# ELU between two matmuls: the Relu on ScalarE is dropped, a two-step clamp is added on VectorE

## What is computed

```python
# 1. gated linear attention, 4 batches x 8 heads, 768 steps, head dim 48
S_re, S_im = a * (S_re, S_im) + (k v^T, 0)      # complex decay a per channel
y[t] = q[t] @ S_re
# 2. MLP with ELU: x is (3072, 384), w_in (384, 2048), w_out (2048, 384)
h = x @ w_in
g = np.where(h > 0.0, h, np.exp(np.minimum(h, 0.0)) - 1.0)
x = g @ w_out
# 3. MLP with a maximum of three: w1, w2, w3 (384, 768), w_fin (768, 384)
out = np.maximum(np.maximum(x @ w1, x @ w2), x @ w3) @ w_fin
```

## Time and profile before

| | |
|---|---|
| time, median of 3 runs | 925.01 us (924.41 to 926.62) |
| time of the profiled execution | 925.01 us |
| span in the profile, first to last instruction | 923.1 us |
| PE busy | 841.4 us, 91% of the span |
| PEld busy | 729.5 us, 79% |
| ACT busy | 478.1 us, 52% |
| DVE busy | 438.9 us, 48% |
| POOL busy | 365.7 us, 40% |
| mean granted TensorE clock | 0.981 |

### The profile page before, as it was taken

The page is one execution under the profiler, slowest core; times in us unless marked ns, Lnnn a source line. Parts: engine busy times, 40 slices in busy tenths (PEclk is TensorE's granted clock), DMA queues, the critical chain, the costliest instruction groups (busy, mean ns, idle before and its releaser), DMA issues.

```text
span 923.1 us, 14390 instructions
## 1 busy us (share of the span) xinstructions
PE 841.4 (91%) x5692; PEld 729.5 (79%) x5692; DVE 438.9 (48%) x606; ACT 478.1 (52%) x709; POOL 365.7 (40%) x272
## 2 busy tenths in 40 slices
PE   0057899999999999999999999999999999999997
PEld 0047799888887888788878888888888889898987
DVE  4857776866666666666757332333112121212120
ACT  6746776777768676868685635642121211211121
POOL 3543654453545454445454423555222131303120
PEclk9987899999999999999999999999999999999999
DMA  5397143636252524353433425002010102000000
GB/s 224 87 277 205 35 135 95 187 103 196 60 169 78 183 73 154 90 172 89 138 112 116 124 82 211 0 27 94 9 60 0 69 1 69 1 35 1 35 0 35
DMA packets 70723, 88.45 MB, mean 96 GB/s; under 512 B 15360, under 2 KB 55296, under 8 KB 70144
## 3 DMA queue, kind: packets, MB, share of 16 engines
q1 hardware_dynamic: 70656, 87.53, 30.4%
HBM read 59.13 MB, written 28.39 MB: 95 GB/s over the span
## 4 chain that ended last, share of the span: by engine, by line
PE 54%; issue 3%; ACT 1%; POOL 1%; POOLq 0%; DVE 0%; ACTq 0%
PE bank L1123 54%; POOL hl L517 1%; ACT t L633 0%; PE bank L1138 0%; ACT ge L633 0%; POOLq L104 0%; ACT gh L633 0%; ACT x2s L633 0%; DVE xl L870 0%; ACT osb L633 0%; POOLq L619 0%; ACTq L729 0%; ACTq L651 0%
## 5 line engine op out<-in xcount | busy, mean ns | idle before, releaser
L517 POOL TENSOR_TENSOR gl<-ge,gh 128x512 fp32r<-128x512 f32 x96 | 128.3, 1337 | 143.1 <-ACT gh L633 143.1
L870 DVE TENSOR_TENSOR hm<-bank,hm 128x512 f32<-128x512 f32 x72 | 49.8, 692 | 226.6 <-PE bank L1123 224.7
L1123 PE MATMUL bank<-xh,wih 128*128 128x512 f32 (+1 forms) x336 | 126.2, 376 | 7.3 <-DVE xl L870 7.3
L1123 PE MATMUL bank<-gh,woh 128*128 128x512 f32 (+1 forms) x336 | 124.1, 369 | 7.2 <-POOL gl L517 4.3
L517 POOL TENSOR_TENSOR hl<-hm,hh 128x512 fp32r<-128x512 f32 x36 | 46.5, 1292 | 205.8 <-ACT hh L633 205.8
L1123 PE MATMUL bank<-xh,wal 128*128 128x512 f32 x324 | 126.1, 389 | 0.0
L1123 PE MATMUL bank<-xl,wah 128*128 128x512 f32 x324 | 126.1, 389 | 0.0
L1123 PE MATMUL bank<-xh,wah 128*128 128x512 f32 x324 | 126.0, 389 | 0.0
L867 DVE SCALAR_TENSOR_TENSOR ge<-ge,bank 128x512 f32<-128x512 f32 x96 | 65.7, 685 | 124.3 <-ACT ge L633 124.3
L1123 PE MATMUL bank<-xh,wil 128*128 128x512 f32 (+1 forms) x336 | 121.9, 363 | 0.0
L1123 PE MATMUL bank<-xl,wih 128*128 128x512 f32 (+1 forms) x336 | 121.7, 362 | 0.0
(11 more groups left out here) (83 smaller groups left out, 1661.8 us busy)
## 6 DMA issues: line engine op xcount, KB each, us to landing
q_cols<-qp SPq DMA_DIRECT2D x24, 384.0 KB, 3.2
k_cols<-kp SPq DMA_DIRECT2D x24, 384.0 KB, 3.0
qt<-q_cols SPq DMA_DIRECT2D x24, 384.0 KB, 3.7
kt<-k_cols SPq DMA_DIRECT2D x24, 384.0 KB, 4.0
vv<-in_v SPq DMA_DIRECT2D x12, 448.0 KB, 4.9
ar<-in_a_re SPq DMA_DIRECT2D x12, 384.0 KB, 3.6
ai<-in_a_im SPq DMA_DIRECT2D x12, 384.0 KB, 4.2
qd<-in_q SPq DMA_DIRECT2D x12, 384.0 KB, 4.6
```

The source lines that it names most:

```text
L517: return nc.gpsimd.tensor_tensor(dst, whole, high.bitcast(f32), ALU.subtract)
L870: return nc.vector.tensor_tensor(dst, a, b, op)
L1123: return nc.tensor.matmul(dst, lhsT, rhs, start=start, stop=stop)
```

## The change

The Relu on ACT goes away, and Exp reads h from PSUM directly. Instead of clamping h before the exponential, the kernel clamps its result: min(exp(h), 1) - 1, a new tensor_scalar on DVE, from SBUF to SBUF in place. The scalar_tensor_tensor behind it then computes max(h, 0) + ge, with the PSUM operand first. ELU comes out the same, since one of the two terms is always zero. The semaphore `below` (ACT on itself) is replaced by `em1` (DVE on itself). All 96 steps change in this way, and nothing else does.

```diff
@@ exp_g(g) on ACT
                 act.wait_ge(up, g + 1)
                 if g >= 2:
                     act.wait_ge(glo, g - 1)
-                func(ge[:, g % 2, :], bank[g % 2][:, :], ACT.Relu, scale=-1.0).then_inc(below, 1)
-                act.wait_ge(below, g + 1)
-                func(ge[:, g % 2, :], ge[:, g % 2, :], ACT.Exp, scale=-1.0).then_inc(exd, 1)
+                func(ge[:, g % 2, :], bank[g % 2][:, :], ACT.Exp).then_inc(exd, 1)
@@ elu_g(g) on DVE
                 dve.wait_ge(exd, g + 1)
-                stt(ge[:, g % 2, :], ge[:, g % 2, :], 1.0, bank[g % 2][:, :], ALU.subtract, ALU.max).then_inc(elu, 1)
+                ts(ge[:, g % 2, :], ge[:, g % 2, :], 1.0, ALU.min, 1.0, ALU.subtract).then_inc(em1, 1)
+                dve.wait_ge(em1, g + 1)
+                stt(ge[:, g % 2, :], bank[g % 2][:, :], 0.0, ge[:, g % 2, :], ALU.max, ALU.add).then_inc(elu, 1)
```

More of the change, by code:

```diff
@@ L236, in build @@
         wohi, wolo = sem("w_out_high"), sem("w_out_low")
-        up, below, exd, elu = sem("up_ready"), sem("below_zero"), sem("exp_ready"), sem("elu_ready")
+        up, exd, em1, elu = sem("up_ready"), sem("exp_ready"), sem("exp_minus_one"), sem("elu_ready")
         ghi, glo, down = sem("elu_high"), sem("elu_low"), sem("down_done")
```

## The result

| | before | after |
|---|---|---|
| median of 4 runs | 924.9 us | 931.5 us (930.5 to 932.2) |
| profiled execution, span | 925.01, 923.1 us | 932.65, 930.9 us |
| ratio, 95% interval | | 1.0067 (1.005 to 1.0085) |

The change makes the kernel slower by 0.67%, 6.2 us of 925 (the two medians of the table lie 6.6 us apart; the ratio is the better number). The forecast was 926.7 us with a range up to 930.5 and "no change" as the likeliest. Both are wrong. The profiled execution of after lies 1.1 us above its median, so differences between the two traces come out a little larger (7.8 us by the spans) than the ratio says.

What follows compares the result with a forecast made beforehand. The prediction took PE to set the time, with the ELU chain costing only where PE waits for it. Its terms, -0.6 - 0.7 + 0.5 + 0.4 + 0.8 + 2.9 + 0.9 - 2.5, gave +1.7 us: 926.7 us, range 922.3 to 930.5.

Steps and rivals of the forecast that it cites:

- st: PE's wait for attention's st at 137 us, behind the ELU of step 8 on DVE: +0.5 us.
- kt: PE's wait at 172 us for kt, a reload of kp behind the ELU of step 11: +0.4 us.
- The price of a clamp: Each added tensor_scalar on DVE: 0.42 us with POOL idle, otherwise ending 0.29 us behind the end of POOL's instruction.
- six places: The places that move by a clamp's wait for POOL: st, kt, and xl at 193, 284, 375 and 466 us.
- ACT's side: Gains from the dropped Relus on ACT, at the kr, gl and x2s waits: -3.8 us.
- x2s: PE's waits for ACT's copy of a tile, which comes up to 0.63 us earlier each: -2.5 us.
- kr: PE's wait of 0.7 us for kr, behind the Exp of step 1 in ACT's queue: -0.6 us.
- gl: PE's wait ended at 109.55 us; sn and gl come 1.26 us earlier: -0.7 us more than kr.
- The chunk's ends: PE's xl waits at 284.37 and 375.66 us; the clamp waits for POOL's gl: two times +1.45, +2.9 us.
- 466: PE's xl wait at 466 us, the ELU coming up during a POOL instruction: +0.9 us.
- The clock rival: Longer xl waits at 284 and 375 us bring falls of TensorE's clock: 930.1 us, chance 0.20.
- The rival with no wait for POOL: The clamp takes 0.42 us for by far most steps, without waiting for POOL: 922.6 us, chance 0.25.

Runs made afterwards that it cites:

- psum_clamp_8_11: The kernel after, with the clamps of steps 8 and 11 as scalar_tensor_tensors that also read h from PSUM; 928.0 us, ratio 1.0036 to before.
- no_clamp: The kernel before with Relu dropped, Exp straight from PSUM and no clamp added (ELU wrong for h above 0); 914.7 us, ratio 0.9881 to before.
- psum_clamp: The kernel after, with all 96 clamps as scalar_tensor_tensors that also read h from PSUM; 927.9 us, ratio 1.0023 to before.
- psum_clamp_half: As psum_clamp, but the clamp works on 256 of the 512 columns, leaving the other half unclamped; 919.9 us, ratio 0.9955 to before.
- after_again: The kernel after, unchanged, measured once more as a control; 931.1 us, ratio 1.0065 to before.
- mixed7: The kernel before, with Relu dropped and the clamp form of psum_clamp in steps 1, 2, 3, 17, 33, 49 and 65 alone; 920.2 us, ratio 0.9958.
- psum_clamp_8: The kernel after, with the clamp of step 8 alone as a scalar_tensor_tensor that also reads h from PSUM; 928.5 us, ratio 1.0026 to before.
- psum_clamp_first16: The kernel after, with the clamp form of psum_clamp in steps 0 to 15 and tensor_scalars in the 80 others; 929.6 us, ratio 1.0057 to before.
- mixed6: The kernel before, with Relu dropped and the clamp form of psum_clamp in steps 2, 3, 17, 33, 49 and 65 alone; 920.9 us, ratio 0.9957.

## Why the prediction was wrong

**The terms for `st` and `kt`.** These are the steps that failed, by 2.7 and 3.5 us. For `st` the prediction had the clamp wait for the one POOL instruction that runs when it comes up, and end at 134.24. It asked of before's trace what POOL was doing at that moment, and not what POOL had ready behind it. The clamp lost a second turn and ended at 137.12. Undoing this one instruction gave 3.8 us back, which shows the cause; in the lag, half of what it gave back was the clock behind the wait, for which the prediction's term had nothing. Of the 3.2 us measured, 2.5 are waiting and 0.6 the clock. For `kt` I took the clamp's own delay only. That delay moved `kp`, an SBUF-to-SBUF instruction that was there already, into POOL's next instruction (+1.1 us) and a chain of two DMAs with it. The longer wait makes 2.3 us of the 3.9, matmuls at half clock behind it 1.6. psum_clamp_8_11 shows that the clamp of step 11 starts this. How much of the 3.9 us is step 8's share isn't separated exactly; with step 8 cured it was 2.7.

**The price of a clamp.** The 0.42 us beside an idle POOL and the tail of 0.29 us behind POOL's end were right (0.41 to 0.43, and 0.28 at step 8), though the working has a slip: 256 columns at 0.56 ns are 0.14 us and not 0.13, which gives 0.40. What was wrong was to price the clamp at six places only and to call all else absorbed. It costs 17.2 us, of which 6.8 by the runs (3.7 by the lags) would be there without any wait for POOL; my terms held 5.5.

**ACT's side.** The four `x2s` waits came out at -2.5 us, as predicted, and the ACT waits are gone from the view. The `kr` term came in after too: the lag falls by 0.75 us at 89 us. But it rises by 0.85 at 99.5 us, so `kr` and `gl` together made +0.35 instead of -1.3: the clamp of step 2 took 2.06 us beside POOL, and `sn` started at 103.31, not 1.26 us earlier than 102.96. no_clamp has -1.94 there. As a whole ACT's side was worth 11.0 us and not 3.8, of which 1.6 are the lower clock at 138 us that no_clamp is spared. I had counted waits by the engine that the view names as the releaser, while waits named after DVE (`st`, two of the `xl`) went away in no_clamp: they stand behind ELU chains, and so behind ACT. That it is the chain in each case is read from the order of the programs and not tested wait by wait.

**The chunk's ends.** +2.9 us was forecast, +0.4 measured. The step that failed is the order of clamp and `gl`. I let DVE come free at the copy's end (282.03), 0.06 us after `gl` had started. But the ELU of before started at 281.95, 0.08 us before the recorded end of the copy and 0.02 before `gl`; the row of the next instruction told who would be first, and I took the other one. A gap of 0.02 us can't bear a term of 1.45, twice. At 466, where POOL was far into its instruction, the term held (+0.7 for +0.9).

**The rivals.** The clock rival had the right mechanism at the wrong place. No fall came at 284 and 375 us, where the waits stayed short. From 84 to 206 us the lower level holds for 20.5 us in after (107.9 to 114.7, 138.6 to 145.4 and 176.2 to 183.0 us) and for 10.2 in before (107.3 to 114.1 and 138.0 to 141.4). It cost after 0.6 us at 138 us and 1.6 at `kt`, some 2 us of the 8.0; 0.7 more up to 177 us fell away again by 187. The window of the last stretch, in after:

```profile
176.00:184.00 8.00, 5.91 (x31) 5.94 (x32) 4.18 (x9) 0.63 (x1) 3.95 (x5) 0.57 0.49 147
```

It cost 1.5 and 1.6 us in psum_clamp and psum_clamp_8_11, at tile 16. There waits of 2.93 and 2.28 us were followed by the lower level, and 1.85 and 1.88 us (in after at 201.38 and in psum_clamp_half) were not. But the length of the wait alone doesn't decide: 2.84 us in after_again at 176.34 and 2.42 us in mixed7 at 170.85 were not followed by it either, and the 2.85 us in layer 3 are followed by 0, 3.4 or 6.8 us of it. The rival with no wait for POOL is what psum_clamp_half built: 922.6 us was its forecast, 919.9 was measured.

**The last 100 us.** +1.2 us was not foreseen, most of it at step 95. Its clamp, at 621.74 us, took 1.13 us beside the `gl` of step 94 (621.30 to 622.59), POOL's `xl` of layer 3 went on behind it, and the last `gl` came at 624.34, to end just ahead of PE's start at 625.67. The chain was read in the trace, but the other traces bear it out: from 613 to 620 us the lag grows by 1.0 us in after_again, psum_clamp_8, psum_clamp_8_11 and psum_clamp_first16, which all have the tensor_scalar in step 95, and by 0.1 at most in no_clamp, psum_clamp and psum_clamp_half, which don't.

**What stays open.** Why DVE lost the second turn at step 8, in both executions, when for example at step 28 of after, with the same two POOL instructions, it got in after the first; what decides how long the lower clock lasts behind a wait; and which of the places between 133 and 202 us takes the loss in a given execution.

Of the two rules of the Trainium skill that the prediction weighed, the first held and the second did not for this change as a whole. "SBUF — State Buffer", section "SBUF: two separate sides", says that the loser of the shared port waits for the winner's whole instruction: the trace agrees, as the clamps that met POOL end about 0.28 us behind the end of its instruction, at step 8 of the second one. "ScalarE: Activation LUTs", section "Rules for kernel authors", wants relu, min and max on VectorE. One instruction is indeed shorter there, 0.42 us beside an idle POOL against 0.60 for the Relu, but dropping the Relu took 11.0 us off and the min on VectorE put 17.2 on.

## What to carry to other kernels

Work that moves from one engine to another is better priced by two kernels that each do half of the change than by the waits of the profile: a wait names the engine that came last, not the one that began the chain. An added instruction that shares a port should be read against the other engine's queue, with all that is ready behind the running instruction, and also against what it pushes. And where an edit helps some steps and hurts others, it can be made in some alone: six steps of 96 gave 0.4% where all 96 cost 0.7%. Before a gain of 1 or 2 us is put down to an edit, the granted clock of both traces should be laid side by side, also in stages that the edit doesn't touch.

## What the runs showed of the hardware

- A DVE instruction from SBUF to SBUF was held up through two POOL instructions in a row: 3.18 us for a work of 0.42, in both executions of after. A scalar_tensor_tensor with one PSUM operand never was: 659 to 691 ns, 192 times.
- POOL waits too: a `gl` of 1.30 us took 1.55 when the clamp had started 0.02 us ahead of it. On DVE not only the clamp is held up: `kp`, a product of two SBUF tensors, 0.56 us undisturbed, took 1.65.
- The two forms of the ELU instruction, 659 to 690 ns with the SBUF operand first and 690 to 695 with the PSUM operand first, differ by 5 ns in the median.
- The same wait of 2.85 us of PE in layer 3 was followed by the full clock (no_clamp, psum_clamp, mixed6), by 3.4 us at the lower level (before, after) or by 6.8 us (psum_clamp_first16, after_again). Between none and 6.8 us lie 2.8 us of time.
